# A fused windowed mix and ELU MLP: second products of two output tiles one pair later, GpSimd's first products in pieces, ScalarE subtracting the one in seven pairs of eight

## The reference

```python
w = weight_gen - np.max(weight_gen, axis=-1, keepdims=True)
w = np.exp(w)
w = w / (np.sum(w, axis=-1, keepdims=True) + 1e-09)
...
out = np.einsum('bshk,bskhg->bshg', w, x_unf)      # 7 taps, 8 heads of 24 channels
...
h = x @ w_in                                        # 192 x 2048
g = np.where(h > 0.0, h, alpha * (np.exp(np.minimum(h, 0.0)) - 1.0))
return (g @ w_out).astype(np.float32)               # 2048 x 192
```

## Time and profile before

| | |
|---|---|
| median of 3 runs | 1230.33 us (1230.3 to 1230.64) |
| the profiled execution, its own time | 1231.57 us |
| its span in the trace | 1229.7 us |
| TensorE busy | 1146.7 us, 93% of the span |
| VectorE busy | 921.1 us, 75% |
| ScalarE busy | 900.0 us, 73% |
| GpSimd busy | 802.4 us, 65% |
| mean granted TensorE clock | 0.991 of full speed |

### The profile page before, as it was taken

How to read it: one execution, slowest core, us unless ns; L and a number is a source line. 1 busy time by engine, 2 the same in 40 slices (tenths; PEclk the granted TensorE clock), 3 DMA queues, 4 the chain that set the end, 5 groups by cost and what they waited for, 6 DMA issues and landing times.

```text
span 1229.7 us, 32008 instructions
## 1 busy us (share of the span) xinstructions
PE 1146.7 (93%) x12848; PEld 1021.8 (83%) x12848; DVE 921.1 (75%) x1431; ACT 900.0 (73%) x1549; POOL 802.4 (65%) x355
## 2 busy tenths in 40 slices
PE   4589999999999999999999999999999999999998
PEld 4478888888888888888888888888888888988887
DVE  7957777777777777777777777777777777777776
ACT  4457777777777777777777777777777777777775
POOL 7775667866667876667876667776667776667410
PEclk9889999999999999999999999999999999999999
DMA  7121333211232211223211233211323311331100
GB/s 217 44 74 40 89 88 88 86 55 33 87 87 87 84 57 33 87 87 87 87 56 31 87 87 87 87 59 30 87 87 87 87 60 31 83 87 51 52 14 14
DMA packets 58774, 88.02 MB, mean 72 GB/s; under 512 B 5224, under 2 KB 38500, under 8 KB 58720
## 3 DMA queue, kind: packets, MB, share of 16 engines
q1 hardware_dynamic: 58720, 87.42, 24.9%
HBM read 62.63 MB, written 24.77 MB: 71 GB/s over the span
## 4 chain that ended last, share of the span: by engine, by line
PE 78%; DVE 10%; ACT 5%; issue 5%; POOL 2%; DMA 0%; DVEq 0%; SPq 0%; POOLq 0%
PE acc L897 40%; PE slot L873 37%; DVE outs L789 5%; DVE g_lo L813 3%; ACT em L642 3%; ACT em L652 2%; POOL prod L453 1%; DMA xwin<-in_x_dram 0%; DVE slot L807 0%; DVE win_lo L760 0%; DVE wout L760 0%; POOL xt_lo L489 0%; POOL prod L470 0%; POOL prod L469 0%; DVE acc L730 0%
## 5 line engine op out<-in xcount | busy, mean ns | idle before, releaser
L897 PE MATMUL acc<-wout,g_hi 64*128 64x384 f32 x4096 | 548.6, 345 | 18.3 <-issue 12.0
L897 PE MATMUL acc<-wout,g_lo 64*128 64x192 f32 x4096 | 380.7, 264 | 44.8 <-DVE g_lo L813 44.4
L897 PEld LDWEIGHTS acc<-wout,g_lo 64*128 64x128 f32 x4096 | 367.0, 186 | 64.0 <-DVE g_lo L813 62.2
L807 DVE SCALAR_TENSOR_TENSOR slot<-em,slot 128x512 f32<-128x512 f32 x384 | 266.3, 695 | 185.9 <-ACT em L652 185.6
L642 ACT ACTIVATE em<-slot 128x512 f32<-128x512 f32 x384 | 227.3, 592 | 205.5 <-PE slot L873 205.5
L897 PEld LDWEIGHTS acc<-wout,g_hi 64*128 64x128 f32 x4096 | 328.7, 188 | 46.0 <-issue 24.4
L489 POOL TENSOR_TENSOR xt_lo<-x_raw,xt 128x512 fp32r<-128x512 f32 x93 | 118.8, 1292 | 358.3 <-ACT xt L635 358.3
L813 DVE TENSOR_TENSOR g_lo<-slot,g_hi 128x512 fp32r<-128x512 f32 x512 | 346.6, 689 | 5.3
L658 ACT ACTIVATE g_hi<-slot 128x512 fp32r<-128x512 f32 x512 | 304.8, 595 | 59.8 <-DVE slot L807 33.9
L453 POOL TENSOR_TENSOR prod<-xwin,probs 128x5376 f32<-128x5376 f32 (+1 forms) x32 | 305.9, 9559 | 7.1 <-POOL probs L448 5.4
L652 ACT ACTIVATE em<-em 128x512 f32<-128x512 f32 x384 | 242.7, 632 | 12.2
(11 more groups left out here) (54 smaller groups left out, 406.2 us busy)
## 6 DMA issues: line engine op xcount, KB each, us to landing
xwin<-in_x_dram SPq DMA_DIRECT2D x29, 960.0 KB, 5.0
x_raw<-turned_dram SPq DMA_DIRECT2D x62, 384.0 KB, 4.7
out_dram<-outs SPq DMA_DIRECT2D x32, 384.0 KB, 2.6
turned_dram<-turned SPq DMA_DIRECT2D x124, 96.0 KB, 2.0
wg<-in_weight_gen_dram SPq DMA_DIRECT2D x32, 112.0 KB, 2.5
xwin<-in_x_dram SPq DMA_DIRECT2D x2, 768.0 KB, 4.6
win_raw<-in_moe_w_in_dram SPq DMA_DIRECT2D x24, 64.0 KB, 3.2
wout_raw<-in_moe_w_out_dram SPq DMA_DIRECT2D x4, 384.0 KB, 4.1
```

Of the source, the lines that this page charges most:

```text
L807: nc.vector.scalar_tensor_tensor(out=slot[slot_of(f)], in0=em[:, f % 2, :], scalar=0.0, in1=slot[slot_of(f)], op0=ALU.min, op1=ALU.max).th ...
L897: last = pe.matmul(acc[t][:, cols], g[rows, f % GBUFS, chunk(t)], wout[rows, f, 0:cols.stop - cols.start], start=(f == 0 and g is g_hi and ...
```

## The change

**Second products.** The steps on tiles 0 and 2 (`EVEN`) stay with their pair; those on tiles 1 and 3 (`ODD`) are made one pair later, between the others: ODD of pair m-1, EVEN of m, ODD of m-1, EVEN of m. The waits for `s_ghi` and `s_split` of pair m now stand in the second step. At a block boundary the ODD steps of pair 7 run in pair 0 of the next block, and after the last block two steps are left over.

```diff
-                steps = [(j, highs + lows_) for j in range(TILES)]
-                pe.wait_ge(s_ghi, b.count(CHUNKS, two + 1))
...
+                earlier = (b, m - 1) if m > 0 else (previous(b), PAIRS - 1)
+                if m == 1:
+
+                    ge(pe, s_out, b.count(TILES))
+                tiles_of(*earlier, ODD[0], b.count(STEPS, rows - 2))
+                if m == 0:
+                    pe.wait_ge(s_out, b.count(TILES, 2 - TILES))
+                pe.wait_ge(s_ghi, b.count(CHUNKS, 2 * m + 2))
+                tiles_of(b, m, EVEN[0], b.count(STEPS, rows))
+                tiles_of(*earlier, ODD[1], b.count(STEPS, rows + 2))
+                tiles_of(b, m, EVEN[1], b.count(STEPS, rows + 4))
```

`tiles_of` holds the 8 matmuls of one step. The buffers of `g_hi` come free later by the same step:

```diff
             done = f // 2 + 1
-            return block.count(STEPS, 2 * TILES * done)
+            return block.count(STEPS, 2 * TILES * done + 2)
```

```diff
         def low_first(m):
 
-            return m >= PAIRS // 2
+            return m == 0
```

```diff
-            products(1, 0, TILES)
+            for t in range(TILES):
+                for taps in ((0, BANK_TAPS), (BANK_TAPS, kernel)):
+                    done = nc.gpsimd.tensor_tensor(prod_of(t, t + 1)[:, taps[0]:taps[1]], taps_of(1, t, t + 1, taps),
+                                                   weights_of(1, t, t + 1, taps), ALU.mult)
+            done.then_inc(s_prod, 1)
```

More of the change, by code:

```diff
@@ L243, in turn_at, with copies_at @@
         def turn_at(b):
-            return (4, (0, 3)) if b.first else (3, (0, 3)) if not b.has_old and b.pair == 0 else (2, (1, 2))
+            return 5 if b.first else 3 if number(b) == 1 else 2
+        def copies_at(b):
+            return {6: (0, PIECES)} if b.first else {5: (0, PIECES)} if number(b) == 1 else {4: (0, 1), 5: (1, PIECES)}
+        LAST_ROW = {t: BLOCKS * STEPS - n for t, n in {2: 5, 0: 4, 3: 1, 1: 0}.items()}
         def by_quad(t):
@@ L277, in taps_of, with weights_of @@
                            ap=[list(t.ap[0]), [d_model, taps[1] - taps[0]], [group, (end - first) * heads], [1, group]])
-        def weights_of(q, first, end):
-            t = probs[:, q, first * HK:]
+        def weights_of(q, first, end, taps=(0, kernel)):
+            t = probs[:, q, first * HK + taps[0]:]
             return bass.AP(tensor=t.tensor, offset=t.offset,
-                           ap=[list(t.ap[0]), [1, kernel], [kernel, (end - first) * heads], [0, group]])
+                           ap=[list(t.ap[0]), [1, taps[1] - taps[0]], [kernel, (end - first) * heads], [0, group]])
         def bank_weights(taps):
@@ L411, in _, with previous @@
                 sp.wait_ge(s_stored[q], 16 * (BLOCKS // 2 + 1))
+        def previous(b):
+            return Block(b.pair, 0) if b.parity == 1 else Block(b.pair - 1, 1)
         def following(b):
@@ L578, in softmaxes @@
         def softmaxes(b):
[L580 to L583, removed]
+            if b.first:
+                return {("max", 0): 2, ("exp", 2): 2, ("sum", 2): 2, ("rec", 4): 2, ("max", 6): 3}
+            late = 7 if number(b) == 1 else 6
             at = {("rec", 0): 2, ("max", 4): 3, ("exp", late): 3, ("sum", late): 3}
+            if number(b) == 1:
+                at = {("exp", 0): 2, ("sum", 1): 2, ("rec", 3): 2, ("max", 4): 3, ("exp", late): 3, ("sum", late): 3}
             return {k: n for k, n in at.items() if number(b) + n < BLOCKS}
@@ L656, in high @@
                 act.wait_ge(s_g, place(b, f))
-                ge(act, s_row, used_count(b, f - GBUFS))
+                if not (b.first and f < GBUFS):
+                    act.wait_ge(s_row, used_count(b, f - GBUFS))
                 nc.scalar.activation(g_hi[:, f % GBUFS, :], slot[slot_of(f)], ACT.Copy).then_inc(s_ghi, 1)
             def body(b):
-                at, pieces = turn_at(b)
                 softmax = softmaxes(b)
@@ L680, in body @@
                         softmax_exp(ahead(b, softmax["exp", m]))
[L681 to L684, removed]
+                    if b.has_next and m in copies_at(b):
+                        high_parts(b, range(*copies_at(b)[m]))
             unrolled_blocks(body)
@@ L827, in body @@
                     softmax_step("rec", m)
-                    if m == turn_at(b)[0] and b.has_next:
+                    if b.first and m - 1 in SPLIT_AT:
+                        low_half(*SPLIT_AT[m - 1])
+                    if m == turn_at(b) and b.has_next:
                         turn(b)
@@ L882, in second_products @@
                 lo = (g_lo, slice(d_model, 2 * d_model))
-                highs, lows_ = ((one, hi), (two, hi)), ((one, lo), (two, lo))
-                steps = [(j, highs + lows_) for j in range(TILES)]
-                pe.wait_ge(s_ghi, b.count(CHUNKS, two + 1))
[L886 to L902, removed]
@@ new lines, in tiles_of @@
+                ge(pe, s_row, rows_done)
+                for n, (f, (g, cols)) in enumerate(((one, hi), (two, hi), (one, lo), (two, lo))):
+                    if n == 2 and tiles == EVEN[0]:
+                        pe.wait_ge(s_split, b.count(CHUNKS, two + 1))
+                    for t, rows in zip(tiles, HALVES):
+                        last = pe.matmul(acc[t][:, cols], g[rows, f % GBUFS, chunk(t)],
+                                         wout[rows, f, 0:cols.stop - cols.start],
+                                         start=(f == 0 and g is g_hi and tiles in (EVEN[0], ODD[0])),
+                                         stop=(f == CHUNKS - 1 and g is g_lo and tiles in (EVEN[1], ODD[1])))
+                        if n == 3:
+                            last.then_inc(s_row, 1)
@@ new lines, in second_products @@
+            def second_products(b, m):
+                rows = 2 * TILES * m - TILES
+                if m == 0 and b.first:
+                    pe.wait_ge(s_ghi, 2)
+                    tiles_of(b, 0, EVEN[0], 0)
+                    tiles_of(b, 0, EVEN[1], 2)
+                    return
+                earlier = (b, m - 1) if m > 0 else (previous(b), PAIRS - 1)
[8 more added lines that the diff above has]
+                tiles_of(b, m, EVEN[1], b.count(STEPS, rows + 4))
```

67 lines of the change are left out of this document (42 added, 25 removed).

## The result

The changed kernel takes **1176.84 us** (median of 4 runs, 1175.76 to 1178.4) against 1230.32 us before (1229.51 to 1230.64): ratio 0.9567, 95% interval 0.9551 to 0.9584. That is 53.5 us; 50.7 were forecast. One later run of the changed kernel, beside experiment 11, took 1321.43 us at a granted clock of 0.772 and is left out everywhere.

A forecast was written before the change was run, and what follows sets the result against it. TensorE bounds the steady part at 4.36 us a pair, and VectorE once in a block. Gains 41.4 + 4.1 + 5.7 - 0.5 = 50.7 us off 1230.33 give about 1180 us, range 1164 to 1199.

The forecast's parts named there:

- The boundary: Block boundaries: TensorE's loss, waiting for VectorE's g_lo, falls from 1.98 to 0.6 us; 30 times, 41.4 us gained.
- A + 5.94: VectorE's second g_lo of pair 0 ready 5.94 us after pair 7's products start (A); TensorE needs it at A + 5.28.
- The echo: Small delay in pair 1 after a boundary, counted with the drawn-out matmul group in the 1.98 us beyond 1.43 idle.
- The form of the pairs: Pairs 4 to 7: ScalarE gets `less_one` in three more pairs a block, VectorE's minimum goes; costed at nothing.
- 0.03 inside: Pair 6, 0.56 us late, has its g_lo at 5.25 against the 5.28 TensorE needs.
- rival 3: ScalarE becomes the one waited for, later loads delaying the transposed block: 0.5 us a block back, 1195 us; chance 0.20.
- The start: Up to block 2: 4.1 us gained from shorter VectorE locks, 5.7 us in block 1, its reciprocal moved to pair 3.
- The lock: VectorE's weight rest (low_half) blocked until GpSimd's block 2 products end; moves from the fourth rest to the fifth.
- rival 1: Start: the fifth weight rest slips in ahead of GpSimd's products, saving 7 and 2 us: 1171 us; chance 0.12.
- The end: After the last pair: two steps more, two reductions beside them; a loss of 0.5 us.
- Rival 2: Block boundary clean, only 0.1 us left: 15 us more gained, 1165 us; chance 0.13.
- Rival 4: Buffer loop, `high` waiting for the third step on the pair before, sets the pitch: slower, 1254 us; chance 0.04.

The follow-up runs named there:

- experiment 11: The changed kernel run again, unchanged, beside two other runs: 1177.16 us (median of three), ratio 0.9561.
- experiment 1: Kernel before with only the new second-product order, spread reductions and single waits for pair 0's input; pair form and start as before: 1181.15 us, ratio 0.9597.
- experiment 6: Changed kernel with VectorE's reciprocal behind the minimum of pair 0, not ahead of it: 1177.49 us, ratio 0.9565.
- experiment 3: Changed kernel with the old form of the pairs (pairs 4 to 7 low-first, pair 0 regular): 1173.18 us, ratio 0.9537.
- experiment 5: Changed kernel with SyncE issuing the window load of x behind the transposed block's DRAM round trip, not ahead: 1170.28 us, ratio 0.9513.
- experiment 9: Changed kernel with the old form of the pairs and the window load behind the round trip: 1172.93 us, ratio 0.9534.
- Experiment 8: Kernel before with only the new form of the pairs (only pair 0 low-first), second products in their old order: 1237.67 us, ratio 1.0061.
- experiment 4: Changed kernel with GpSimd waiting for all five weight rests before it begins block 2's products: 1166.43 us, ratio 0.9483.
- experiment 10: Changed kernel with g_hi buffers waited for one step longer (all four steps on the pair before, not three): 1176.23 us, ratio 0.9532.
- experiment 2: Changed kernel with GpSimd's products and pair sums of block 1 whole again, not in pieces: 1178.09 us, ratio 0.9573.

## Why the prediction was right

**The boundary.** Right in mechanism, too small in size by 0.16 us a block net. Forecast 30 x (1.98 - 0.6) = 41.4 us; measured 44.7 for 29 blocks and 2.0 for the last boundary. The loss left over was put at 0.6 and is two things: 0.20 at the boundary and 0.22 at pairs 5 to 7, of which the sum had only the first. That the net came so near is luck in part: 0.4 too much in one term and 0.22 too little in another half cancel. My sum for VectorE, A + 5.94, came out at A + 5.32. Two of its terms were too large: the 0.2 for a late pair 7 was 0 (VectorE ended it at A + 0.33, as the rows gave), and whole durations were added where instructions overlap at their ends by about 0.1 each. By the sum's own rule A + 5.32 would leave 0.04, and 0.20 was lost: the matmul group that is drawn out around the wait, about 0.16, was in the 1.98 and not in the 0.6. The echo, which the prediction put in pair 1, stands two pairs on and is gone too. Experiment 1 shows that the order with the spread reductions removes the wait whatever the form of the pairs, and 6 that the 0.2 left is the reciprocal.

**The form of the pairs, costed at nothing.** This is the step that failed, if by little. Pair 6 was counted 0.03 inside, and so it was as long as x_raw was there. I had named the later window loads only in rival 3, at a chance of 0.20 and 0.5 us a block; they came, at 0.22. The part of the change that was to cost nothing costs 3.7 us (experiment 3), and with the window load moved it brings 2.7 (experiments 5 and 9). Experiment 8 shows the cover: without the step on the earlier pair the same form costs 0.49 a block at those pairs, and with it, where nothing waits for x_raw (experiment 5), 0.

**The start.** Forecast 4.1 + 5.7 = 9.8 us up to block 2, measured 9.9. The sum is nearer than its terms: up to the second products of the first block's pair 7 (76.03 before, 70.99 after) 5.0 were gained and not 4.1, and in block 1 4.9 and not 5.7. The lock moved to the fifth rest as written: GpSimd began at 45.00 (45.6 forecast), the rest took 10.13 us. The rule of the Trainium skill ("SBUF — State Buffer", "Who interferes with whom"), that the one which issues second is blocked until the first has finished, agrees with it, and with experiment 4, where GpSimd is held back and no rest takes over 1.5 us. VectorE reached it at 45.38 and not 47.9: it had gained 5 us on the first pairs, not 2.5. So rival 1 was nearer than I put it, and the side on which it fell was decided by 0.4 us; the 1166.0 us of experiment 10 may be the other side. Its price is right: experiment 4 gives 10.4 us for 9. The clock did not fall again behind 64 us, in contrast to the earlier trace rows. All parts of the start together are worth 8.0 us (experiments 1 and 3), the pieces 1.3 of them (experiment 2); the other 1.9 of the 9.9 came with the order, under which block 2 begins at 113.69 in experiment 1. Within the 8.0, the softmax steps a pair later, with which the reciprocal's 4.5 us went, and the rests at the start of a pair were not taken apart.

**The end.** Loss forecast 0.5 us. The last block gained 1.2 in all, of which 1.98 is its boundary, so 0.8 was lost.

**The rivals.** Rival 2 (a clean boundary) is experiment 6's boundary, and rival 3 came half. Rival 4, the buffers, falls with experiment 10: a release 0.57 us later changes nothing.

## What to carry to other kernels

A consumer that waits for the newest result can be given a step on the previous one to do first; here one step of 0.57 us, moved ahead of the wait, and the two reductions of 0.97 us that it allowed to be put off took away 1.64 of 1.98 us a block (experiment 1). Before an engine is given more work because it has room on average, look at the one place where it is already late, and at what SyncE issues ahead of the transfer that it waits for there. And when a repair shows no gain though its wait is gone, as in experiment 6, look for the next wait in the same block before giving it up.

## What the runs showed of the hardware

VectorE's subtraction of two SBUF tensors took 1.0 to 1.9 us beside instructions of GpSimd of at most 1.9 us each, and 10.13 us behind one of 9.71. GpSimd's work in pieces took longer: four pair sums of 576 elements 6.31 us where the whole took 5.15 in the kernel before. At the 0.18 us that the prediction reads for each further instruction that is 0.5 of the 1.2 us; the rest may be VectorE's subtraction between them, which is argued and not shown. And a transfer of 96 KB issued 1.2 us behind one of 960 KB landed after 4.1 us, in place of 2.0 when it was issued 3.9 us behind.
